# Six pairs of a last chunk's second down product as plain fp32, with the fraction from a Newton step

## The reference

```python
def _moe2_ref(x, w_in, w_out, a, b):
    h = x @ w_in                                     # 192 -> 2048
    h2 = h * h
    h3 = h2 * h
    P = a[0] + a[1] * h + a[2] * h2 + a[3] * h3
    Q = 1.0 + np.abs(b[0]) * np.abs(h) + np.abs(b[1]) * h2
    g = P / (Q + 1e-06)
    return g @ w_out                                 # 2048 -> 192
```

## Time and profile before

| | us |
|---|---|
| median of three runs | 1311.95 (1310.11 to 1312.54) |
| profiled execution | 1310.99 |
| its span, first to last instruction | 1309.2 |
| TensorE / DVE / ScalarE / GpSimd busy | 1259.6 / 1252.4 / 1105.6 / 658.4 |
| mean granted TensorE clock | 0.99 of 2.4 GHz |

### The profile page before, as it was taken

One profiled execution on the slowest core, in us unless ns is written; L12 is line 12 of the kernel. 1 busy time (PEld: TensorE's weight loads), 2 busy tenths in 40 slices (PEclk: granted clock), 3 DMA queues, 4 the chain that ended last, 5 costly groups with the idle time before them and its releaser, 6 DMA issues.

```text
span 1309.2 us, 16870 instructions
## 1 busy us (share of the span) xinstructions
PE 1259.6 (96%) x5440; PEld 1022.5 (78%) x5440; DVE 1252.4 (96%) x1201; ACT 1105.6 (84%) x1278; POOL 658.4 (50%) x337
## 2 busy tenths in 40 slices
PE   5989999999999999999999999999999999999866
PEld 4868888788888888888887888878888888888654
DVE  7779999999999999999999999999999999989998
ACT  6579888888988888898988888888898888888773
POOL 1425555455556456456455455555455545554433
PEclk9989999999999999999999999999999999999898
DMA  8000000000000000000000100000000000000000
GB/s 225 25 1 21 2 13 21 9 25 0 25 7 12 20 5 27 0 12 20 8 24 0 32 0 12 20 8 24 0 21 12 12 20 0 20 1 13 1 13 12
DMA packets 15960, 23.66 MB, mean 18 GB/s; under 512 B 2240, under 2 KB 10048, under 8 KB 15936
## 3 DMA queue, kind: packets, MB, share of 16 engines
q1 hardware_dynamic: 14160, 21.30, 5.7%
q10 hardware_dynamic: 1776, 2.06, 0.7%
HBM read 13.13 MB, written 6.29 MB: 15 GB/s over the span
## 4 chain that ended last, share of the span: by engine, by line
PE 87%; DVE 8%; issue 3%; ACT 1%; POOL 1%; DMA 0%; SPq 0%; DVEq 0%; POOLq 0%; ACTq 0%
PE up_ps L304 11%; PE up_ps L305 10%; PE up_ps L306 10%; PE up_ps L307 10%; PE up_ps L308 10%; PE acc_main L311 7%; PE acc_main L312 7%; PE acc_main L314 7%; PE acc_tail L313 7%; PE acc_tail L315 7%; DVE denom L1201 1%; DVE numer L1164 1%; DVE denom L1191 1%; DVE denom L1154 1%; DVE numer L1172 1%
## 5 line engine op out<-in xcount | busy, mean ns | idle before, releaser
L983 POOL TENSOR_TENSOR frac_low<-denom,seed 128x1024 fp32r<-128x1024 f32 x126 | 377.3, 2994 | 526.9 <-DVE denom L1201 524.9
L974 POOL TENSOR_TENSOR gated_low<-gated,gated_high 128x512 fp32r<-128x512 f32 x192 | 264.1, 1392 | 109.6 <-ACT gated_high L658 109.6
L304 PE MATMUL up_ps<-x_high,up_high 128*128 128x512 f32 x640 | 254.8, 398 | 34.6 <-DVE x_low L1233 15.9
L305 PE MATMUL up_ps<-x_high,up_low 128*128 128x512 f32 x640 | 251.7, 393 | 0.0
L306 PE MATMUL up_ps<-x_low,up_high 128*128 128x512 f32 x640 | 251.4, 393 | 0.0
L307 PE MATMUL up_ps<-x_tail_high,up_tail 128*128 128x512 f32 x640 | 251.0, 392 | 0.0
L308 PE MATMUL up_ps<-x_tail_low,up_tail 128*128 128x512 f32 x640 | 250.8, 392 | 0.0
L678 ACT ACTIVATE numer<-up_ps,coef 128x1024 f32<-128x1024 f32 x128 | 154.4, 1206 | 34.2 <-PE up_ps L308 30.7
L1164 DVE TENSOR_TENSOR numer<-up_ps,numer 128x1024 f32<-128x1024 f32 x128 | 156.2, 1220 | 24.6 <-ACT seed L669 18.6
L669 ACT ACTIVATE seed<-up_ps,coef 128x1024 f32<-128x1024 f32 x128 | 142.6, 1114 | 41.3 <-PE up_ps L308 27.9
L304 PEld LDWEIGHTS up_ps<-x_high,up_high 128*128 128x128 f32 x640 | 121.5, 190 | 69.5 <-DVE denom L1154 21.4
(11 more groups left out here) (87 smaller groups left out, 2254.7 us busy)
## 6 DMA issues: line engine op xcount, KB each, us to landing
x_raw<-x_chunks SPq DMA_DIRECT2D x16, 393.0 KB, 3.1
out_chunks<-out_main SPq DMA_DIRECT2D x16, 256.0 KB, 2.1
tail_twice<-conv SPq DMA_DIRECT2D x60, 64.0 KB, 2.0
out_chunks<-tail_part SPq DMA_DIRECT2D x16, 128.0 KB, 2.3
numer<-w_out SPq DMA_DIRECT2D x1, 1536.0 KB, 8.5
seed<-w_out ACTq DMA_DIRECT2D x1, 1152.0 KB, 14.5
denom<-w_in SPq DMA_DIRECT2D x2, 512.0 KB, 4.7
denom<-w_gate SPq DMA_DIRECT2D x1, 576.0 KB, 5.8
```

Source lines behind the costliest of these rows:

```text
L304: nc.tensor.matmul(acc, up_high[:, cols], x["high"][:], start=True, stop=False)
L305: nc.tensor.matmul(acc, up_low[:, cols], x["high"][:], start=False, stop=False)
L974: nc.gpsimd.tensor_tensor(gated_low[:, b], gated[:, b], gated_high[:, b], ALU.subtract).then_inc(gated_low_done, 1)
L983: nc.gpsimd.tensor_tensor(ring(frac_low, j, 2, LOW_RING), ring(denom, j), ring(seed, j), ALU.mult).then_inc(frac_low_done, 1)
```

## The change

Pairs 1 to 6 of the last chunk (`WHOLE`) are no longer split. Pairs 0 and 7 and all pairs of other chunks stay as they are.

- **Weights:** the twelve tiles of `w_out2` that these pairs need are loaded again as they are, by six transfers on SP's queue, into `gated` (four pairs) and `conv` (two). SP waits for the last uses of both buffers first; the transfers stand ahead of the last two stores.
- **TensorE:** `down_whole` takes the place of `down_fraction` or `down_last`: per tile one fp32 matmul with 128 weight columns and one with 64.
- **Fraction:** ScalarE adds 1 + eps to the denominator (`raise_denominator`), log and exp give the seed s of it, GpSimd makes Q s in place (`unity`), DVE (Q s - 2) s in place of the seed (`inverse`), which is the negative of a Newton step, and (numer - a0) times that (`whole_fraction`). So `slope_minus` and `cubic_minus` work with the negated coefficients `minus_a`, which ScalarE makes once at the start. `product`, `rest` and `low_fraction` or `last_low` fall away for these pairs.
- **Waits:** counts of the semaphores that these pairs don't signal any more are lowered (`parted`). `magnitude` of pair n waits for `whole_fraction` of n-4, and `slope` of n for TensorE to be done with pair n-4, where that pair is a whole one.
- **Order:** the drain is written anew on every engine. ScalarE takes exp(-4) ahead of log(-3), and round_x1_main ahead of copy_x1_part; DVE takes split_x1_main and sum_x1_tail ahead of denominator(-1); TensorE has down_fraction(-2) ahead of up_h(3) and down_fraction(0) ahead of up_h(5).

```diff
+WHOLE = (1,2,3,4,5,6)
...
+        def parted(count):
+            if not isinstance(count, int):
+                return count
+            return count - sum(1 for n in WHOLE if n < count - (chunks - 1) * pairs2)
+        def numer_read(count):
+            n = count - 1 - (chunks - 1) * pairs2 if isinstance(count, int) else None
+            return (down2_done, 2 * count) if n in WHOLE else (rest_done, parted(count))
+        def seed_read(count):
+            n = count - 1 - (chunks - 1) * pairs2 if isinstance(count, int) else None
+            return (whole_done, whole(n)) if n in WHOLE else (frac_low_done, parted(count))
...
+            sp.wait_ge(gated_high_done, chunks * tiles1)
+            sp.wait_ge(gated_low_done, chunks * tiles1)
+            sp.wait_ge(x0_main_high, chunks)
+            sp.wait_ge(x0_main_low, chunks)
+            sp.wait_ge(tail_in, 64 * (chunks - 1))
+            for n in WHOLE:
+                rows = w_out2[2 * n * P:2 * (n + 1) * P, :]
+                sp.dma_start(whole_down2(n), rows.rearrange("(t p) n -> p t n", p=P)).then_inc(whole_in, 16)
             store(chunks - 2)
             store(chunks - 1)
...
+            def down_whole(i, w, p):
+                count, j = pair_of(i, w, p)
+                n = j // 2
+                if n == WHOLE[0]:
+                    pe.wait_ge(whole_in, 16 * len(WHOLE))
+                pe.wait_ge(whole_done, whole(n))
+                for a in range(2):
+                    weights, frac = whole_down2(n)[:, a], ring(numer, j + a, 1)
+                    nc.tensor.matmul(acc2_main[:], weights[:, 0:P], frac, start=False, stop=False)
+                    nc.tensor.matmul(acc2_tail[0:tail], weights[:, P:d_model], frac,
+                                     start=False, stop=False).then_inc(down2_done, 1)
...
             up_h(*late(2))
+            down_fraction(*late(-2))
             up_h(*late(3))
-            down_fraction(*late(-2))
             down_fraction(*late(-1))
             up_h(*late(4))
+            down_fraction(*late(0))
             up_h(*late(5))
-            down_fraction(*late(0))
-            down_fraction(*late(1))
+            down_whole(*late(1))
+            down_whole(*late(2))
             up_h(*late(6))
             up_h(*late(7))
-            down_fraction(*late(2))
-            down_fraction(*late(3))
-            down_fraction(*late(4))
-            down_fraction(*late(5))
-            down_last(*late(6))
+            down_whole(*late(3))
+            down_whole(*late(4))
+            down_whole(*late(5))
+            down_whole(*late(6))
             down_last(*late(7))
...
+            def raise_denominator(i, w, p):
+                count, j = pair_of(i, w, p)
+                act.wait_ge(denom_done, count)
+                den = ring(denom, j)
+                nc.scalar.activation(den, den, ACT.Identity, bias=1.0 + RATIONAL_EPS).then_inc(raised_done, 1)
+            def log_raised(i, w, p):
+                _, j = pair_of(i, w, p)
+                act.wait_ge(raised_done, whole(j // 2))
+                nc.scalar.activation(ring(seed, j), ring(denom, j), ACT.Ln).then_inc(log_done, 1)
...
+            def unity(i, w, p):
+                count, j = pair_of(i, w, p)
+                pool.wait_ge(seed_done, count)
+                den = ring(denom, j)
+                nc.gpsimd.tensor_tensor(den, den, ring(seed, j), ALU.mult).then_inc(unity_done, 1)
...
+            def inverse(i, w, p):
+                _, j = pair_of(i, w, p)
+                dve.wait_ge(unity_done, whole(j // 2))
+                nc.vector.scalar_tensor_tensor(ring(seed, j), ring(denom, j), 2.0, ring(seed, j),
+                                               ALU.subtract, ALU.mult).then_inc(inverse_done, 1)
+            def whole_fraction(i, w, p):
+                count, j = pair_of(i, w, p)
+                dve.wait_ge(soft_act, 3)
+                dve.wait_ge(inverse_done, whole(j // 2))
+                dve.wait_ge(numer_done, count)
+                nc.vector.scalar_tensor_tensor(ring(numer, j), ring(numer, j),
+                                               minus_a[:, 0:1], ring(seed, j),
+                                               ALU.add, ALU.mult).then_inc(whole_done, 1)
```

More of the change, by code:

```diff
@@ L213, in build, with whole_down2 @@
         first_col = {"gate": 0, "val": d_ff1, "in": 2 * d_ff1}
+        assert len(WHOLE) <= 6 and 8 * d_model == G_TILES * T and 4 * d_model == BLOCKS * HALF
+        def whole_down2(n):
+            place = whole(n) - 1
+            if place < 4:
+                held = gated[:].rearrange("p b n -> p (b n)")
+            else:
+                held, place = conv[:].rearrange("p b n -> p (b n)"), place - 4
+            return held[:, place * 2 * d_model:(place + 1) * 2 * d_model].rearrange("p (t n) -> p t n", t=2)
         split_order = [("gate", 0), ("val", 0), ("gate", 1), ("val", 1), ("out1", 0), ("in", 0), ("in", 1), ("out2", 0)]
@@ L335, in down_fraction @@
                 if count is not None:
-                    after(pe, frac_low_done, count)
+                    after(pe, frac_low_done, parted(count))
                     if j == 0:
@@ L560, in _ @@
             nc.scalar.activation(tap_w[:], logits[:], ACT.Exp).then_inc(soft_act, 1)
+            nc.scalar.activation(minus_a[:], coef[:, 0:4], ACT.Copy, scale=-1.0).then_inc(soft_act, 1)
             def round_weights_main(name, n):
@@ L667, in magnitude @@
                     act.wait_ge(h_ready, 2 * count)
-                    after(act, frac_low_done, count - RING)
+                    after(act, *seed_read(count - RING))
                     nc.scalar.activation(ring(seed, j), up_bank(i, w, 2 * p, 2), ACT.Abs,
@@ L898, in _ @@
             log_table()
+            exp(*late(-4))
             log(*late(-3))
-            exp(*late(-4))
+            magnitude(*late(-2))
             round_gated(chunks - 1, 3, 1)
             slope(*late(-2))
+            exp(*late(-3))
             round_gated(chunks - 1, 3, 2)
-            magnitude(*late(-2))
-            exp(*late(-3))
             magnitude(*late(-1))
@@ L918, in _ @@
             slope(*late(0))
-            slope(*late(1))
+            slope_minus(*late(1))
+            magnitude(*late(1))
             square(*late(0))
-            magnitude(*late(1))
             log(*late(0))
@@ L1046, in _ @@
             low_fraction(*late(0))
-            low_fraction(*late(1))
-            low_fraction(*late(2))
-            low_fraction(*late(3))
-            low_fraction(*late(4))
-            low_fraction(*late(5))
+            unity(*late(1))
+            unity(*late(2))
+            unity(*late(3))
+            unity(*late(4))
+            unity(*late(5))
+            unity(*late(6))
         @block.vector
@@ L1408, in _ @@
             rest(*late(-4))
+            split_x1_main(chunks)
+            sum_x1_tail(chunks)
             denominator(*late(-1))
[L1410 to L1411 removed]
             split_x1_tail(chunks)
@@ L1420, in _ @@
             rest(*late(-2))
+            quadratic(*late(1))
             denominator(*late(0))
-            quadratic(*late(1))
-            cubic(*late(1))
+            cubic_minus(*late(1))
             product(*late(-1))
```

133 lines of the change are left out of this document (75 added, 58 removed).

## The result

The changed kernel took 1306.86 us (median of 7 runs, 1306.56 to 1308.22) beside 1311.35 for the kernel before on the same chip (7 runs): ratio 0.9969, with a 95% interval of [0.9958, 0.9979], so faster by 0.2 to 0.4%. Run again later beside the kernel before it took 1307.99 against 1310.98: 0.9977 [0.9968, 0.9986]. The forecast was 1308.4, 3.5 less than before; the two measurements are 4.5 and 3.0 less. The profiled execution took 1307.26 with a span of 1305.1, against 1310.99 and 1309.2.

What follows compares the result with a forecast made beforehand. DVE was taken to bound the drain: -8.0 work, +4.5 waits, -1.1 GpSimd conflict, -0.5 early moves and rounding, +1.6 TensorE's end gave -3.5 us, from 1311.95 to a median of 1308.4; range 1305.4 to 1313.6.

Steps and rivals of the forecast that it cites:

- DVE's work, -8.0: Drain on DVE: six whole pairs save 6.8 us and last_low of pair 6 goes, 1.14, together -8.0 us.
- Waits at denominator(3), denominator(7), inverse(4): DVE in the drain: three waits of 1.15, 1.15 and 2.20 us carry a growth of DVE's waits by 4.5 us.
- The early moves, 0.4: Start of the drain: earlier x1 splits, with exp(-4) ahead of log(-3), bring 0.4 us, 0.5 with rounding.
- last_low(7) at -5.1: DVE's last product of the drain ends at 1298.7 instead of 1303.8: -8.0 + 4.5 - 1.1 - 0.5 = -5.1 us.
- A fp32 matmul at 0.91: TensorE, whole pairs: a plain fp32 matmul costs four full-clock passes of 0.227, 0.91 us, a pair 3.63.
- TensorE's end, +1.6: End of the drain: after 3.5 us idle, pair 6 runs at 1.2 GHz, ending at 1301.6 instead of 1300.0, +1.6 us.
- unity on GpSimd, one meeting of six: GpSimd in the drain: unity takes 2.4 us, and one of six meets a DVE instruction with two SBUF inputs.
- unity on DVE weighed at about +1 beside before: Alternative placing in the drain: 6.8 us more on DVE, one wait of 2.2 less, the change at about +1.
- (b): Rival: TensorE bounds the end through dearer fp32 matmuls; gain gone at 1.38 us each, +6.5 at 1.71; chance 0.12.
- (c): Rival: GpSimd sets the pace, unity taking 3.0 to 3.4 us; chance 0.22 partly, within 0.2%, and 0.06 wholly, slower.
- (a): Rival: the clock holds in the last gap or fp32 matmuls are cheaper; -5.1 us, 1306.8; chance 0.25.
- (d): Rival: freed time turns into 2 to 3 us more waits in the drain; 1311, chance within the 0.22 of (c).

Runs made afterwards that it cites:

- bank_wait: Changed kernel with up_h(6) waiting for denominator(4) and up_h(7) for denominator(5), not the other way round; 1307.67 us, ratio 0.9971 to the kernel before.
- bank_wait_before: Kernel before, with up_h of pair n in the drain waiting for the denominator of pair n-2; 1311.37 us, ratio 0.9998 to the kernel before.
- front_only: Kernel before with only the changed kernel's new order of early instructions, up to about 1237 us; 1311.12 us, ratio 0.9999 to the kernel before.
- no_raise: Changed kernel without the six raise_denominator instructions, log adding 1 + eps as its bias; 1308.31 us, ratio 0.9977 to the kernel before.
- unity_dve: Changed kernel with GpSimd's six unity products done by DVE, each ahead of its inverse; 1315.88 us, ratio 1.0038 to the kernel before.
- changed_again: Changed kernel run once more unedited, giving its second profile; 1307.99 us, ratio 0.9977 to the kernel before.

## Why the forecast held, step by step

- **DVE's work, -8.0: right.** The page has 8.4 less. inverse takes 1.22 us, as a product does, and not the 1.27 that was taken for it; but whole_fraction(1) needs the inverse(1) just before it and starts 1.30 behind it (1260.43 to 1261.73), where 1.20 to 1.25 was taken. Behind whole_fraction the next one starts 1.21 later. The 1.1 us that the last product of before lost to GpSimd fell away too: product(7) now takes 1.23.
- **Waits at denominator(3), denominator(7), inverse(4): right** in place, releaser and size: 1.07, 1.08, 2.16 for 1.15, 1.15, 2.20.
- **The early moves, 0.4 (with rounding 0.5) on DVE's side: right as a start, not quite as a gain.** up_h(0) came 0.5 earlier; 0.2 to 0.5 of it arrived.
- **last_low(7) at -5.1: too much, by 1.35 in the first profile and 0.6 in the second.** The term at fault is that of the waits. Over the stretch that ends at last_low(7), from 10.03 us behind the gate on (that is from 1222 us on in the kernel before), DVE's busy time fell by 9.0 and 9.1, where -8.0 and -1.1 were forecast; its idle time grew from 1.8 to 7.1 and 6.4, +5.2 and +4.6, where +4.5 less the 0.5 of the early moves was forecast. The rules of "The kernel before" let up_h(6) start when denominator(4) is done; the trace has it behind denominator(5). From the end of denominator(4) to last_low(7) it placed 27.8; the profiles have 28.8 and 27.9. With the clock held the late up_h(6) costs 0.1 at most (27.9, and 27.9 in bank_wait too). What makes the 1.0 is the clock: with it low, up_h(6) and (7), magnitude(6), exp(5) and unity(5) came late, and inverse(5) waited 0.76. The other 0.4 to 0.5 lie ahead of denominator(4), where the first quadratic of the last chunk waited 0.96 and 1.13 us for slope, while the clock was at 0.85 and 0.78 (1230 to 1245 us). In bank_wait, with 0.89 there, that wait was 0.64. The prediction took its share of slow matmuls there from one profile.
- **A fp32 matmul at 0.91: too cheap.** It costs 1.06 or 1.00 us, 4.12 a pair and not 3.63. With 0.227 a pass those are 4.7 and 4.4 passes. The Trainium skill, FP8 and Floating Point Precision, section TensorE Precision Notes, gives true fp32 four passes through the array; this trace has 10 to 17% more than four of its fp32r passes.
- **TensorE's end, +1.6: +0.44.** The gap ahead of pair 6 was smaller than placed. Pairs 3 to 5 ran back to back until 1292.7, so pair 6 came 1.55 us behind them and not 3.5, and at full clock. Three pairs at 4.12 in place of 3.63 make 1.5 of that; in the first profile the slow up_h(6) and (7) ahead of them add some (in the second the gap is 2.22, and the clock held there too). What is left is a plain bound by TensorE: pair 6 and ten passes of pair 7 end 0.44 later behind last_low(7) than the four passes of before. The premise that a gap of nearly 3.4 us is what makes the clock fall, and a shorter one spares it, holds by half: behind every gap of over 3.1 us in these drains the clock was low or fell, but it also fell behind shorter ones. Even the gap of 2.78 us behind which it held comes again, ahead of the same instructions, in bank_wait_before (2.78) and front_only (2.77), and there the matmuls behind it started 0.43 us apart. In the kernels where pair 6 did run at the low clock, the end grew by 2.0 (4.47 and 4.49 against 2.52), so the 1.6 had about the right size for a case that didn't come in either profile of the changed kernel.
- **So the sum was right by two errors of opposite sign**: +1.35 or +0.6 of missing gain on DVE, -1.2 at the end. That the total fits to 0.2 and 0.6 us (3.3 and 4.1 for 3.5) is in part luck. That DVE's work falls by about 8, that over half of it comes back as waits, and where the three largest of them stand, was worked out and came so.
- **The raises at nothing: right** (37.91, and 37.96 without them). That a raise dearer by 0.2 would move the end by 0.2 isn't tested, and the 0.37 us that square(5) waits behind raise(4) and log(4) speaks against it at that link. **SP's loads at nothing: right**: six transfers of 192 KB, issued at 1221.7 to 1224.7, landed in 2.9 (median of four) and 3.6 us (of two), some 35 us ahead of their use.
- **unity on GpSimd, one meeting of six: nearly.** Four took 2.35 to 2.41 us and two were held up, 2.92 and 2.66, begun while DVE was in whole_fraction (1261.73 to 1263.01 in DVE's lines above); nothing waited for those two. Timeline of GpSimd in the changed kernel:

```profile
1262.33 2.92 POOL L1078 TENSOR_TENSOR denom<-denom,seed 128x1024 f32<-128x1024 f32 x1 [2.27 <-ACT seed L789]
1267.61 2.66 POOL L1078 TENSOR_TENSOR denom<-denom,seed 128x1024 f32<-128x1024 f32 x1 [2.37 <-ACT seed L789]
1273.84 2.41 POOL L1078 TENSOR_TENSOR denom<-denom,seed 128x1024 f32<-128x1024 f32 x1 [3.56 <-ACT seed L789]
```

- **unity on DVE weighed at about +1 beside before: too low.** It is +3.9 in the drain and +4.6 in time. The weighing gave back the whole 2.2 of one wait and kept the end as it was; neither held. The Trainium skill, GPSIMD Engine Reference, section Engine selection, would put these products on VectorE; by these runs that costs 7 to 8 us of the drain, because VectorE is the engine that is full.
- **The rivals.** (b), TensorE as the bound, is what the last link now is, at a size of 0.44; its break-even of 1.38 us a matmul was not reached. (c), GpSimd setting the pace, did not come. (a) had the end's clock right and its DVE time wrong. (d), 2 to 3 us more of waits than placed, came only in part, as the 1.35 and 0.6 above.

Left open: why the clock fell at up_h(6) in some profiles and not in others, how often it does so in unprofiled runs, and what makes the first 100 us vary by a microsecond. That bank_wait protects the time is likely (there the array goes into up_h(6) without standing still for long, 0.6 us at most, and in the three profiles of the two kernels that have it the clock held, against two of five with the crossed wait) but not shown, since its time can't be told from the changed kernel's. Of the ten times of no_raise four stand at 1309.7 to 1309.8, the profiled one among them, and none between these and 1308.5; that would fit a fall at pair 6 in four of ten executions, but only one of them has a profile.

## What to carry to other kernels

Cutting a full engine's work pays only in part in a drain that is written by hand: here, of 9 us less of DVE's work about 5 came back as waits. The three largest could be placed beforehand from the old trace; those that hang on the clock could not. The next gain came from order (inverse(4) behind quadratic(6)), not from less work. Before a difference of under 1 us between two profiles is explained, profile the unedited kernel again and compare from an anchor inside the trace: one such repeat took back a cause that an experiment had seemed to show. Cheaper matmuls on an engine that isn't the bound can bring nothing: with one pass in place of fp32 the array stood idle more, its clock was lower, and the time was the same. Dearer ones are no safeguard either: in no_raise and unity_dve the last fp32 pair ran at the lower clock.

## What the runs showed of the hardware

- A plain fp32 matmul of 512 columns costs 1.06 us start to start with 128 weight columns and 1.00 with 64, at full clock, as two records; it scales with the columns (2 x 256 cost the same). An fp32r pass costs 0.227. At the lower clock the one with 128 weight columns costs 2.01 (no_raise and unity_dve); no run has one with 64 wholly at that clock.
- How long the array stood still does not by itself say whether the clock falls. Behind 2.78 us it held in the kernel before and was low in bank_wait_before, ahead of the same instructions. It held after 2.22 (changed_again) and 2.17 (bank_wait) and was low after 2.24 (no_raise). After 1.86 to 1.89 it fell, about a microsecond later, in three profiles of five, in one of two of the same kernel.
- A GpSimd product of two SBUF tensors that begins while DVE is in an instruction with two SBUF inputs takes longer by about what is left of that instruction: 2.92 for 2.35 us with 0.68 left of whole_fraction(1), 2.66 with 0.43 left of whole_fraction(2). So the meetings were mild here, 0.3 to 0.6 us on two of six products.
